# An attention, expert and dense kernel on one core: state read on quarters of the array, both halves of the turned weights on ScalarE, and loops with their last round written out

## The reference, cut to what matters

```python
# attention, for each batch and head: x is 512 x 64, state is 32 x 64
a     = softmax(x @ state.T / 8);   xread = a @ state      # token read, 512 x 64
a2    = softmax(state @ x.T / 8);   sread = a2 @ x         # state read, 32 x 64
rows  = concat(xread, sread), heads side by side           # 544 rows of 512 per batch
# experts: each row goes to one of 8
logits = normalized(rows) @ normalized(emb).T / tau
e      = argmax(logits);  gate = max of softmax(logits)
out    = gate * (relu(rows @ w1[e]) @ w2[e])
# dense
h = out @ w_in;  r = relu(h);  result = (s * r * r + b) @ w_out
```

## Time and profile before

| | us |
|---|---|
| median of 3 runs (1397.58 to 1402.76) | 1397.78 |
| the profiled execution, its own time | 1393.17 |
| its span, first to last instruction | 1391.1 |
| PE busy | 1345.2 (97%) |
| DVE busy | 645.1 (46%) |
| ACT busy | 506.7 (36%) |
| POOL busy | 192.6 (14%) |

### The profile page before, as it was taken

One profiled execution on the slowest core, in us unless ns is written; L12 is line 12 of the kernel. 1 busy time (PEld: TensorE's weight loads), 2 busy tenths in 40 slices (PEclk: granted clock), 3 DMA queues, 4 the chain that ended last, 5 costly groups with the idle time before them and its releaser, 6 DMA issues.

```text
span 1391.1 us, 23074 instructions
## 1 busy us (share of the span) xinstructions
PE 1345.2 (97%) x6908; PEld 1105.3 (79%) x6909; DVE 645.1 (46%) x1648; ACT 506.7 (36%) x951; POOL 192.6 (14%) x341
## 2 busy tenths in 40 slices
PE   7998899999999999999999999999999999999996
PEld 5776688877788778779888888888888888888884
DVE  5898546666645664757323223232232332322322
ACT  4885335545434643544222222222222222222221
POOL 2236322221222122200001001000010010100101
PEclk9999999999999999999999999999999999999998
DMA  8755313553512451240100001001010010100000
GB/s 252 224 145 193 115 57 103 180 184 108 184 49 68 149 185 49 71 170 9 48 0 31 32 0 62 0 15 47 0 62 0 0 62 0 62 0 0 31 0 31
DMA packets 71938, 103.61 MB, mean 74 GB/s; under 512 B 40424, under 2 KB 41048, under 8 KB 70624
## 3 DMA queue, kind: packets, MB, share of 16 engines
q1 hardware_dynamic: 57824, 72.16, 15.8%
q0 software_dynamic: 8448, 20.40, 4.4%
q10 hardware_dynamic: 5632, 10.60, 2.0%
HBM read 71.81 MB, written 31.34 MB: 74 GB/s over the span
## 4 chain that ended last, share of the span: by engine, by line
PE 81%; DVE 7%; issue 4%; DMA 2%; DVEq 2%; POOL 1%; ACT 1%; ACTq 0%; POOLq 0%; SPq 0%
PE bank_a L1570 26%; PE bank_n L1589 14%; PE bank_tt L1589 12%; PE bank_a L1492 11%; PE bank_n L1525 10%; DMA xg<-x_tok,g_idx 2%; PE bank_tt L1505 1%; PE bank_n L1423 1%; DVEq L363 1%; POOL slot_tab L497 1%; PE bank_tt L1294 1%; PE bank_a L1275 1%; DVE w_in_lo L1044 1%; DVEq L366 1%; PE bank_l L1556 1%
## 5 line engine op out<-in xcount | busy, mean ns | idle before, releaser
L1212 DVE TENSOR_TENSOR sq<-rel 128x512 f32<-128x512 f32 (+1 forms) x144 | 95.4, 663 | 478.4 <-ACT rel L817 478.4
L817 ACT ACTIVATE rel<-bank_a 128x512 f32<-128x512 f32 (+1 forms) x144 | 82.8, 575 | 534.9 <-PE bank_a L1570 534.9
L1570 PE MATMUL bank_a<-y_hi,w_in_hi 128*128 128x512 f32 (+1 forms) x576 | 218.1, 379 | 1.5 <-DVE y_lo L1204 1.4
L1570 PE MATMUL bank_a<-y_hi,w_in_lo 128*128 128x512 f32 (+1 forms) x576 | 217.6, 378 | 0.0
L1570 PE MATMUL bank_a<-y_lo,w_in_hi 128*128 128x512 f32 (+1 forms) x576 | 217.6, 378 | 0.0
L582 POOL DMA_INDIRECT out_rows<-w_raw,out_id x34 | 32.9, 968 | 714.5 <-DVE w_raw L1223 652.1
L1570 PEld LDWEIGHTS bank_a<-y_hi,w_in_hi 128*128 128x128 f32 x576 | 108.4, 188 | 23.0 <-DVE y_lo L1204 1.8
L1570 PEld LDWEIGHTS bank_a<-y_lo,w_in_hi 128*128 128x128 f32 x576 | 108.4, 188 | 20.6 <-issue 0.2
L1570 PEld LDWEIGHTS bank_a<-y_hi,w_in_lo 128*128 128x128 f32 x576 | 108.4, 188 | 19.9
L1525 PE MATMUL bank_n<-w_hi,hid_hi 128*128 128x512 f32 x296 | 115.5, 390 | 1.5 <-DVE hid_lo L1069 1.5
L1525 PE MATMUL bank_n<-w_hi,hid_lo 128*128 128x512 f32 x296 | 115.4, 390 | 0.0
(11 more groups left out here) (237 smaller groups left out, 2136.3 us busy)
## 6 DMA issues: line engine op xcount, KB each, us to landing
w_raw<-in_moe_w SPq DMA_DIRECT2D x16, 2048.0 KB, 10.6
moe_tok<-yg ACTq DMA_DIRECT2D x38, 272.0 KB, 2.1
x_tok<-x_rows SPq DMA_DIRECT2D x8, 1088.0 KB
y_rows<-moe_tok SPq DMA_DIRECT2D x8, 1088.0 KB, 5.3
x_m<-in_x SPq DMA_DIRECT2D x7, 1024.0 KB, 9.4
win_raw<-in_moe_w_in SPq DMA_DIRECT2D x8, 512.0 KB, 10.7
w_raw<-in_moe_w_out SPq DMA_DIRECT2D x1, 4096.0 KB, 16.2
slot_tab<-w_lo SPq DMA_DIRECT2D x2, 1152.0 KB, 6.6
```

The costliest lines, as they stand in the source:

```text
L817: nc.scalar.activation(rel[:, k, 0:cols], ps_g[k][:, 0:cols], ACT.Relu).then_inc(rel_ready, 1)
L1212: nc.vector.tensor_tensor(sq[:, 0:cols], rel[:, k, 0:cols], rel[:, k, 0:cols], ALU.mult).then_inc(sq_ready, 1)
L1570: last = nc.tensor.matmul(ps_g[n % 2][:, 0:cols], w[:, wc], a[:, c, 0:cols], start=(c == 0 and w is w_in_hi and a is y_hi), stop=(c == DC ...
```

## The change

Part by part:
- The state read issues one product per head, 32 x 64, on one quarter of the array's columns each: 32 products of 64 columns per batch in place of 16 of 128.
- `a1_evac` of both halves is ScalarE's; VectorE's is gone.
- In batch 0 the turning of the scores moves ahead of the state transposes, `embed_states` moves behind the state read, VectorE evacuates the turned states (`evac_st`) behind its subtraction, and ScalarE takes the first two x tiles behind the token exponential.
- GpSimd's second early gather is issued two table writes earlier.
- In the experts' loop VectorE's `gate_scale` is cut into `gate_norm` (8 steps), ahead of `next_w2`, and `gate_root` (the other 9), behind it. ScalarE's `store` moves behind its `next_w2`.
- The loops end one round earlier (`prev`, a second number read from the table), and the last round is written out without the parts for a tile after the last.

```diff
 def state_read(bb):
     for jj in range(2):
         for t in range(TPB):
-            for par in range(2):
-                p = slice(HP * par, HP * par + HP)
-                j = 2 * jj + par
-                last = nc.tensor.matmul(bank_r[p, jj * P:(jj + 1) * P], a2_n[:, t, jj * P + HP * par:jj * P + HP * par + HP],
-                                        x_m[bb % 3][:, t, j * P:(j + 1) * P], start=(t == 0), stop=(t == TPB - 1))
+            for q in range(P // NS):
+                p = slice(NS * q, NS * q + NS)
+                c = (q % 2) * DH
+                h = jj * (P // NS) + q
+                last = nc.tensor.matmul(bank_r[p, jj * P + c:jj * P + c + DH], a2_n[:, t, jj * P + NS * q:jj * P + NS * q + NS],
+                                        x_m[bb % 3][:, t, h * DH:(h + 1) * DH], start=(t == 0), stop=(t == TPB - 1))
 # ScalarE
 def a1_evac(bb):
-    act.wait_ge(a1_tr, 2 * bb + 1)
-    if bb >= 1:
-        act.wait_ge(xread_done, TPB * bb)
-    nc.scalar.activation(a1_t[:, 0, :], bank_a[0][:], ACT.Copy).then_inc(a1_ready, 1)
+    for jj in range(2):
+        act.wait_ge(a1_tr, 2 * bb + jj + 1)
+        if jj == 0 and bb >= 1:
+            act.wait_ge(xread_done, TPB * bb)
+        nc.scalar.activation(a1_t[:, jj, :], bank_a[jj][:], ACT.Copy).then_inc(a1_ready, 1)
...
-    store(g)
     next_w2(g)
-with act.Fori(2, last) as g:
+    store(g)
+with act.Fori(2, prev) as g:
     tile(g)
+hidden(last)
+gate_soft(last)
+result(prev)
+hidden_hi(last)
+next_w2(prev)
+store(prev)
 # VectorE
-    if i >= 1:
-        a1_evac(i - 1)
-    else:
+    if i == 0:
         embed_turned()
-        for k in range(1, B // 2):
-            evac_st(k)
...
-    gate_scale(g + 2)
+    gate_norm(g + 2)
     next_w2(g)
+    gate_root(g + 2)
-with dve.Fori(2, last) as g:
+with dve.Fori(2, prev) as g:
     tile(g)
+gate_final(last)
+hidden_lo(last)
+next_w2(prev)
 # TensorE
-with pe.Fori(2, last_g) as g:
+with pe.Fori(2, prev) as g:
     tile(g)
+turn_hidden(prev)
+up(last_g)
+down(prev)
 turn_hidden(last_g)
 # GpSimd
-write_slots(SOON)
+write_slots(SOON, end=TPB - 1)
 gather(1)
+write_slots(SOON, first=TPB - 1)
```

More of the change, by code:

```diff
@@ L99, in attention_moe_ffn @@
         gi = sb(top, "gi", [P, 2], i32)
-        used = sum(-(-n // 32) * 32 for n in (4 * P, 4 * P, 2 * P, 2 * P, 4 * PAIRS * E, 4 * (3 * NSLOT + 1), 4 * IDW, 4, 4 * NSLOT, 4 * NSLOT,
+        used = sum(-(-n // 32) * 32 for n in (4 * P, 4 * P, 2 * P, 2 * P, 4 * PAIRS * E, 4 * (3 * NSLOT + 2), 4 * IDW, 4, 4 * NSLOT, 4 * NSLOT,
                                               4, 4, 4, 4 * TROWS, 4 * E, 4 * E, 32, 8))
@@ L443, in _ @@
             sp.sem_inc(load_turn, 1)
-            sp.wait_ge(gate_sq, last + 3)
+            sp.wait_ge(gate_sq, last + 2)
             sp.sem_inc(load_turn, 1)
@@ L491, in _, with write_slots @@
             nc.gpsimd.memset(late[:, 0:EARLY], 0.0).then_inc(tab_zero, 1)
-            def write_slots(bb):
+            def write_slots(bb, first=0, end=TPB + 1):
                 pool.wait_ge(pos_ready, bb + 1)
-                for t in range(TPB + 1):
+                for t in range(first, end):
                     n = P if t < TPB else NS
@@ L560, in _ @@
             gather(4)
-            with pool.Fori(2, last) as g:
+            with pool.Fori(2, prev) as g:
                 gather(g + 3)
                 result_ids(g)
+            result_ids(prev)
             result_ids(last)
@@ L679, in _ @@
                 nc.scalar.activation(e1[:], e1[:], ACT.Exp, scale=-1.0).then_inc(e1_done, 1)
+                if i == 0:
+                    for j in range(2):
+                        x_evac(1, j)
                 if i + 1 < B:
@@ L848, in emb_link, with rsqrt_seed, rsqrt_rounds @@
                 dve.wait_ge(emb_step, n_emb[0])
-            def rsqrt_steps(link, y, t, n2, iy, it):
+            def rsqrt_seed(link, n2, iy, it):
                 link(nc.vector.tensor_single_scalar(it, n2.bitcast(i32), 1, ALU.arith_shift_right))
                 link(nc.vector.tensor_scalar(iy, it, -1.0, RSQRT_SEED, ALU.mult, ALU.add))
-                for _ in range(3):
+            def rsqrt_rounds(link, y, t, n2, rounds):
+                for _ in range(rounds):
                     link(nc.vector.scalar_tensor_tensor(t, y, n2, y, ALU.mult, ALU.mult))
@@ L1007, in _ @@
                     .then_inc(sh_done, 1)
+                if i == 0:
+                    for k in range(1, B // 2):
+                        evac_st(k)
                 dve.wait_ge(e2_done, 2 * i + 2)
@@ L1077, in gate_link, with gate_norm @@
                     dve.wait_ge(gate_step, GATE_STEPS * g + n_gate[0])
+                return n_gate, gate_link
+            def gate_norm(g):
+                n_gate, gate_link = gate_linker(g, 0)
                 dve.wait_ge(gate_lg, g + 1)
@@ L1083, in gate_scale, with gate_root @@
                 gate_link(nc.vector.tensor_copy(gc[:, 0:1], n2s[:, ds(g, 1)]))
[L1084 removed]
+                rsqrt_seed(gate_link, gc[:, 0:1], gc[:, 4:5].bitcast(i32), gi[:, 0:1])
+                rsqrt_rounds(gate_link, gc[:, 4:5], gc[:, 5:6], gc[:, 0:1], 1)
+                assert n_gate[0] == NORM_STEPS
+            def gate_root(g):
+                n_gate, gate_link = gate_linker(g, NORM_STEPS)
+                rsqrt_rounds(gate_link, gc[:, 4:5], gc[:, 5:6], gc[:, 0:1], 2)
                 gate_link(nc.vector.tensor_tensor(gc[:, 6:7], gc[:, 0:1], gc[:, 4:5], ALU.mult))
@@ L1088, in gate_scale @@
                 assert n_gate[0] == GATE_STEPS - 1
+            def gate_scale(g):
+                gate_norm(g)
+                gate_root(g)
             def gate_final(g):
@@ L1438, in _ @@
                     scores(i)
+                if i >= 1:
+                    turn_a1(i - 1)
+                    turn_rows(i - 1)
+                turn_scores(i)
                 if i == 0:
@@ L1442, in _ @@
                         st_transpose(k)
-                else:
-                    turn_a1(i - 1)
-                    turn_rows(i - 1)
-                turn_scores(i)
                 turn_e2(i)
-                if i == 0:
-                    embed_states()
-                else:
+                if i >= 1:
                     row_logits(i - 1)
@@ L1455, in _ @@
                 state_read(i)
+                if i == 0:
+                    embed_states()
                 if i + 1 < B:
```

32 lines of the change are left out of this document (18 added, 14 removed).

## The result

| | median us | lowest to highest | runs |
|---|---|---|---|
| kernel before | 1399.88 | 1397.14 to 1403.60 | 20 |
| changed kernel | 1404.91 | 1399.54 to 1410.56 | 20 |

The ratio is 1.0038, 95% interval 1.0029 to 1.0046: the change costs 5.3 us (4.1 to 6.4). That is inside what I called no change (0.5%, 7.0 us) and 4.2 us above the forecast of 1400.7. Their difference of 15.8 us is therefore three times the real one, and where it comes from is the first thing to sort out.

What follows compares the result with a forecast made beforehand. TensorE's own row and its short waits were taken as the bound; 1.7 - 0.5 + 0.1 + 3.4 - 1.8 = +2.9 on 1393.17 gave 1396.1, plus 4.6 carried over made 1400.7 us, range 1391 to 1409.

Steps and rivals of the forecast that it cites:

- The state read: Attention's state read on four quarters: claimed bound by number of records, 2.04 us against 1.97, rounded to 0 change.
- rival 1: State read: quarters run side by side, up to 0.98 us less per read, about 5.2 saved, 1395.5 us; chance 0.13.
- the nearest row: Profile row of embed_states: 64 records of 8 columns in 2.04 us, 32 ns each, taken as the new read's cost.
- that row simply shifts: TensorE's third-gather wait, ending at 152.93, was said to move only with the start of the table writes at 119.11.
- The second copy: Attention: ScalarE's added copy delays exponentials 0.4 us, +1.7 over batches 2 to 6; VectorE's dropped copy gives -0.5.
- Batch 0 and the table: Batch 0's new order: 0, between -1 and +1; table writes and moved second gather: 0, the wait reappearing later.
- The change of expert: Experts' loop: w_lo wait goes, xg_lo comes 0.48 us later at each of seven changes, +3.4 us.
- the way back: The loop's way back on VectorE at a change of expert, 0.48 us, formerly hidden beside splits, now exposed.
- the sum: All terms together: +2.9 us against the profiled execution's 1393.17, giving 1396.1 before the carry-over to the median.
- The exit: Loop's end: y_lo wait goes (-1.4) and four unused turned tiles go (0.4); together -1.8 us, between -1.2 and -2.6.
- The next thing late is the low part of the last hidden rows: At the loop's exit, what would be late once the y_lo wait is gone; said to keep its place.
- The anchor: Base time: profiled execution 1393.17 us, plus 4.6 carried over to the median of the runs shown, 1397.78.

Runs made afterwards that it cites:

- e6: Changed kernel with the experts' loop part undone (VectorE's linked steps whole and ahead of the w2 split, ScalarE's store ahead of its split): 1.0004 of the kernel before, +0.6 us.
- e7: Kernel before with the quartered state read, ScalarE's second copy, the earlier gather and the new exit, without the new order of batch 0: ratio 1.0001.
- e1: Kernel before with only the state read on quarters of the array, 64 records instead of 32: ratio 0.9980, -2.8 us.
- e2: Kernel before with the state read on quarters and both copies of the turned token weights on ScalarE: ratio 0.9974, -3.6 us.
- e4: Kernel before with only the second gather moved ahead of the last two table writes of its batch: ratio 0.9983, -2.4 us.
- e3: Kernel before with only the loop's part: VectorE's linked steps cut around its w2 split, ScalarE's store behind its split: ratio 1.0048, +6.7 us.
- e8: Kernel before with only VectorE's half of the loop's part, the gate's linked steps cut around the w2 split: ratio 1.0042, +5.9 us.
- e9: Kernel before with only ScalarE's half of the loop's part, its w2 split ahead of its store: ratio 0.9999.
- e12: Changed kernel with gate_root moved behind xg_lo of the next round: 0.9957 of the kernel before, -6.0 us.

## Why the prediction was right, and where it was not

**The state read: the step was wrong, rival 1 was right.** I took the nearest row, 32 ns a record, and said that the number of records counts. A record took 17 ns (1.10 us for 64); the read is 0.87 us shorter. Rival 1 had this with 0.98, and its limit of 12.45 us a batch was right: 12.35 to 12.56 in the kernels without stalls (e6, e7), where I had 13.29. That the forecast of the attention came near all the same is luck. I and rival 1 both let a batch's change of length reach the end, and it doesn't: on a chip without stalls the shorter batches are 2.98 us ahead at the last scores, and at the loop 0.42 are left of the whole lead (e7). On one with stalls the read alone is worth 2.8 us (e1). Rival 1's price of 5.2 us is in neither. I had noticed that `xg` of the third tile is late, and said "that row simply shifts"; the first gather, which had no wait before, was the one to ask about.

The Trainium skill, TensorEngine Tiling (Array Packing), Theoretical Speedup, which has up to two times for 64 and up to four for 32, held here: from two parts of the array to four the read went from 1.97 to 1.10 us, near half. Its Instruction Overhead, by which I estimated 1.6 us, did not hold for these records; the measurement decides.

**The second copy.** The exponential comes 0.48 us later, as forecast (0.4). Its price of 1.2 us is not shown: e2 is 0.8 us below e1, and the interval of each reaches some 2 us to each side.

**Batch 0 and the table.** 0, as forecast (e6 against e7), and in the way forecast: in the changed kernel's profile the scores of batch 1 start 1.27 us later (28.21 against 26.94), and that batch takes 12.12 us instead of 13.90. The new 3 us wait of the moved gather, and the writes it delays, I had not seen; I had counted the transfers between two points, not the wait that moves along with a gather. Alone the moved gather even gains 2.4 us (e4). Nor does GpSimd write without pause until the third gather lands, as I had read the earlier trace rows: in the kernel before its last write starts at 139.13, and then it waits 4.87 us for the writes to land before it can read the table.

**The change of expert: right in mechanism, one term missed.** The wait for `w_lo` went, `xg_lo` became the wait, two tiles take 27.09 us (forecast 26.9). `xg_lo` is 0.68 us later, not 0.48: the way back shows 0.32 of its 0.48, and the idle time ahead of the split, with the table reads, is 1.89 us where it was 1.46, which I had as a bound only. 7 x 0.68 = 4.8 us. The missed term is TensorE's clock, to which my sum gave nothing: the wait grew from 0.18 to 1.8 us, and behind four of seven such waits the products ran at the lower level, 1.4 to 1.6 us each. The loop from first tile to last is 10.1 us longer in the profiles (453.85 against 443.76); over the runs it costs 6.7 us at the median (e3), where I had 3.4. That is enough for the error of the sum, which was +2.9 forecast and +5.0 between the medians. The changed kernel spreads over 11 us and the one before over 6.5. Stretches at the lower level that come in some executions and not in others would do this, but that isn't shown.

**The exit.** -0.6 measured, -1.1 by the profile, -1.8 forecast. The wait and the turned tiles went as said. "The next thing late is the low part of the last hidden rows" was wrong: it is `g_lo`, 0.70 us.

**The anchor.** Adding the sum to the profiled execution and carrying over the 4.6 us to the median was right, and needed. But that median was of 3 runs, 1397.78; over 20 runs it is 1399.88. So 2.1 us of the 4.2 by which the result lies above the forecast come from the anchor, and only the other 2.1 from the sum. The profiled execution had none of the stalls that other kernels with its attention show on a slower chip (e3, e4). Who compares the two profiles directly reads 15.8 us, of which 6.8 lie ahead of the loop (its first tile at 172.84 against 166.02), and puts on the account of the change what kernels with the attention of before show on other chips by themselves.

## What to carry to other kernels

A wait of TensorE that grows can cost more than its length, as it did at four changes of seven here: ask of every edit that makes one wait longer, even if it removes another, whether the sum in one place goes past what was there. When steps are only moved around a long block on an in-order engine, compare the end of the whole row and not its start. And what is saved in a stage counts only as far as the next thing that this stage does not make: follow the first transfer that another engine's writes must precede. Take the anchor from as many runs as the difference needs, and look in both profiles for a lead that is there before the changed code runs.

## What the runs showed of the hardware that was not expected

- Float32 products of 32 stationary and 64 streamed columns, on four quarters in turn, went at 17 ns a record: below the 32 ns of the earlier trace rows. The Trainium skill, TensorE: Matmul & The Clock Gate, under "Wait — 56ns, not 53.3ns?", says that start-to-start never drops below about 25 ns; in this trace it does, where neighbouring records use different quarters.
- Waits of 1.5 to 1.8 us were enough for TensorE's clock to be at 1.2 GHz behind them in four changes of seven (changed kernel twice, e3, e8), never behind the waits of 0.2 to 0.4 us in the loops of the kernel before and of e9 and e12. Which of the seven it was changed from execution to execution, and not with the length of the wait (1.64 us ahead of a slow one, 1.79 ahead of a fast one).
- The same kernel took 1391.4, 1400.7 and 1403.4 us on three chips. In profiles of kernels with the attention of before on the slower two, batches 4 to 6 take 14.3 to 14.6 us on one (e3, e4) and 13.4 to 17.0 on the other (e8, e9) instead of 12.9, with a copy that starts late on turned tiles whose records had ended. Why these copies start late is open: the profile names no releaser, and no run here was made for it.
